# Attention scores as four 64 by 64 products a unit over 192 of 256 keys, with one bias table for all later query tiles

## The reference

```python
scores = scale * np.matmul(q, k.transpose(0, 1, 3, 2))     # 2 batches, 8 heads, 768 rows, 64 wide
is_global = pos[None, :] < int(n_global)                   # 8 keys
is_local = (rel >= 0) & (rel < int(n_local))               # 96 keys
...
scores = np.where(keep, scores + bias, -1000000000.0)
a = np.exp(scores - np.max(scores, axis=-1, keepdims=True))
a = a / (np.sum(a, axis=-1, keepdims=True) + 1e-09)
return np.matmul(a, v)
```

## Time and profile before

| | us |
|---|---|
| the profiled execution, its device time | 368.6 |
| its span (first to last instruction on the core) | 366.7 |
| outside the span | 1.9 |
| median of the three timed executions | 368.89 |

### The profile page before, as it was taken

One profiled execution on the slowest core, in us unless ns is written; L12 is line 12 of the kernel. 1 busy time (PEld: TensorE's weight loads), 2 busy tenths in 40 slices (PEclk: granted clock), 3 DMA queues, 4 the chain that ended last, 5 costly groups with the idle time before them and its releaser, 6 DMA issues.

```text
span 366.7 us, 6163 instructions
## 1 busy us (share of the span) xinstructions
PE 358.0 (98%) x2272; PEld 325.0 (89%) x2272; DVE 215.3 (59%) x574; ACT 177.9 (49%) x450; POOL 91.2 (25%) x168
## 2 busy tenths in 40 slices
PE   7999999999999999999999999999999999999994
PEld 3568898999899999999989999998999999998883
DVE  7886787777777498699785861114853444440000
ACT  3887667677766489663463732113653111112221
POOL 7899786444444200000030300003400000000000
PEclk9999999999999999999999999999999999999999
DMA  7961322333314024213000000000341000002222
GB/s 219 395 218 66 95 95 86 122 133 114 114 45 150 10 65 138 86 59 114 2 0 0 3 0 0 2 32 14 113 131 44 0 2 0 2 0 88 86 87 92
DMA packets 12085, 27.70 MB, mean 76 GB/s; under 512 B 1552, under 2 KB 3984, under 8 KB 12048
## 3 DMA queue, kind: packets, MB, share of 16 engines
q1 hardware_dynamic: 11760, 27.10, 21.8%
q10 hardware_dynamic: 288, 0.13, 0.2%
HBM read 24.08 MB, written 3.15 MB: 74 GB/s over the span
## 4 chain that ended last, share of the span: by engine, by line
PE 93%; DVE 4%; DMA 1%; issue 1%; ACT 0%; POOL 0%; DVEq 0%
PE bank L1570 20%; PE bank L1572 20%; PE bank L1571 20%; PE bank L1534 18%; PE bank L1513 5%; PE bank L1489 5%; PE bank L1444 5%; DVE p_sb L1063 2%; DMA counts<-in_n_keys 1%; DVE xT L1085 0%; DVE denom L1072 0%; DVE table L1040 0%; ACT p_sb L730 0%; DVE pt_sb L1080 0%; ACT out_sb L801 0%
## 5 line engine op out<-in xcount | busy, mean ns | idle before, releaser
L1534 PE MATMUL bank<-xT,w_hi 128*128 128x384 f32 x256 | 69.5, 345 | 0.0
L630 POOL TENSOR_SCALAR p_sb<-p_sb,denom 128x256 f32<-128x256 f32 (+1 forms) x96 | 47.1, 505 | 42.0 <-DVE denom L1074 42.0
L730 ACT ACTIVATE p_sb<-p_sb,row_min 128x256 f32<-128x256 f32 (+1 forms) x96 | 46.3, 486 | 20.9 <-DVE row_min L1063 20.6
L1534 PEld LDWEIGHTS bank<-xT,w_hi 128*128 128x128 f32 x256 | 45.8, 188 | 0.3 <-issue 0.2
L1534 PE MATMUL bank<-xT,w_lo 128*128 128x384 f32 x128 | 44.0, 344 | 0.0
L1570 PE MATMUL bank<-g_hi,w_hi 128*128 128x386 f32 (+1 forms) x128 | 43.3, 338 | 0.0
L1572 PE MATMUL bank<-g_hi,w_lo 128*128 128x386 f32 (+1 forms) x128 | 43.2, 337 | 0.0
L1571 PE MATMUL bank<-g_lo,w_hi 128*128 128x386 f32 (+1 forms) x128 | 43.1, 337 | 0.0
L1100 DVE SCALAR_TENSOR_TENSOR c_sb<-h_sb,conv_sb,c_sb 128x382 f32<-128x382 f32 (+1 forms) x64 | 41.7, 652 | 2.3
L1063 DVE CUSTOM_DVE_ANT_0 p_sb<-bank,table 128x256 f32<-128x256 f32 (+1 forms) x96 | 32.9, 398 | 13.1 <-PE bank L1444 12.7
L651 POOL TENSOR_SCALAR rstd<-mean_var 128x1 f32<-128x1 f32 x12 | 4.7, 391 | 129.2 <-DVE mean_var L1128 129.2
(11 more groups left out here) (96 smaller groups left out, 776.7 us busy)
## 6 DMA issues: line engine op xcount, KB each, us to landing
stage<-in_weights SPq DMA_DIRECT2D x17, 512.0 KB, 3.2
v_sb<-in_v SPq DMA_DIRECT2D x8, 390.0 KB, 3.8
k_sb<-in_k SPq DMA_DIRECT2D x8, 384.0 KB, 3.3
out_dram<-out_sb SPq DMA_DIRECT2D x12, 256.0 KB, 2.2
q_sb<-in_q SPq DMA_DIRECT2D x13, 192.0 KB, 2.4
v_sb<-in_v SPq DMA_DIRECT2D x6, 260.0 KB, 3.2
k_sb<-in_k SPq DMA_DIRECT2D x5, 256.0 KB, 2.7
stage_late<-in_weights SPq DMA_DIRECT2D x2, 512.0 KB, 11.0
```

Of the source, the lines that this page charges most:

```text
L630: nc.gpsimd.tensor_scalar(probs_h, probs_h, denom[:, u % SLOTS, h:h + 1], 1.0, ALU.mult, ALU.mult).then_inc(scaled, 1)
L730: nc.scalar.activation(p_sb[:, u % SLOTS, h, 0:n], p_sb[:, u % SLOTS, h, 0:n], ACT.Exp, bias=row_min[:, u % SLOTS, h:h + 1], scale=-1.0, a ...
L1534: last = nc.tensor.matmul(h_bank(j)[:, 0:C], w, x, start=r == 0, stop=r == F1_GROUP - 1)
```

## The change

Each product is cut into two halves of 64 queries. The keys of a unit now stand as 96 before the tile, 32 first, 128 own, so the first half needs columns 0 to 191 and the second 64 to 255: 192 each. The four products of a unit take the four quarters of the array (two heads by rows, two halves by columns). At `t` = 0 all 128 keys are kept for both halves. The columns that a half leaves out keep what the bank held; the table gives them a value that hides them, and at the start PE writes zeros to the six banks of scores in place of six of the seven warming products. Since `t` = 1 now has its keys in the order of later tiles, one table part serves them all: 384 columns in place of 640, built by DVE alone. The host packs keys and values in the new order (same bytes). DMAs of a second path for wider bands change too; that path does not run with these inputs.

```diff
-WARM = (7, 3, 3, 3)
-TW = 5 * P
+WARM = (1, 3, 3, 3)
+TW = 3 * P
...
-AT_T1, AT_LATER, AT_T0 = 0, 2 * P, 4 * P
+AT_T0, AT_LATER = 0, P
+HALF = P // 2
+NEAR = WK + GK + HALF
...
+SCORE_BANKS = (0, 1, 2, 5, 6, 7)
...
-            nc.gpsimd.iota(rel[:, AT_T0:TW], [[-1, P]], base=0, channel_multiplier=1, **iota).then_inc(consts, 1)
-            nc.gpsimd.iota(rel[:, AT_T1:AT_LATER], [[-1, 2 * P]], base=P, channel_multiplier=1, **iota
...
+            tiles = rel[:, 0:2 * P].rearrange("p (t n) -> p t n", t=2)
+            nc.gpsimd.iota(tiles[:, :, 0:WK], [[P, 2], [-1, WK]], base=-GK, channel_multiplier=1, **iota
...
+            nc.gpsimd.iota(tiles[:, :, WK:P], [[S, 2], [-1, GK]], base=0, channel_multiplier=1, **iota
...
+            nc.gpsimd.iota(rel[:, 2 * P:TW], [[-1, P]], base=0, channel_multiplier=1, **iota).then_inc(consts, 1)
...
-            later = table[:, AT_LATER:AT_T0]
-            pool.wait_ge(tables, COUNT_STEPS)
-            nc.gpsimd.tensor_scalar(later, rel[:, AT_LATER:AT_T0], count_f[:, 1:2], 1.0, ALU.is_ge, ALU.mult
-                                    ).then_inc(later_table, 1)
-            pool.wait_ge(later_table, 1)
-            nc.gpsimd.tensor_tensor(later, later, behind[:, AT_LATER:AT_T0], ALU.add).then_inc(later_table, 1)
...
-            def build_table(at_col, width):
-                cols, near = slice(at_col, at_col + width), table[:, at_col:at_col + GK]
-                link(nc.vector.scalar_tensor_tensor(table[:, cols], rel[:, cols], nl, behind[:, cols], ALU.is_ge,
-                                                    ALU.max))
-                link(nc.vector.tensor_tensor(near, near, reach[:], ALU.min))
+            def build_table():
+                link(nc.vector.scalar_tensor_tensor(table[:], rel[:], nl, behind[:], ALU.is_ge, ALU.max))
+                for at_col in (AT_T0, AT_LATER):
+                    near = table[:, at_col + WK:at_col + P]
+                    link(nc.vector.tensor_tensor(near, near, reach[:], ALU.min))
...
-                at_col = (AT_T0, AT_T1, AT_LATER)[min(t, 2)]
+                at_col = AT_T0 if t == 0 else AT_LATER
...
-            near = table[:, AT_LATER:AT_LATER + GK]
-            dve.wait_ge(later_table, 2)
-            link(nc.vector.tensor_tensor(near, near, reach[:], ALU.min))
...
-            def score(u, h):
+            def score(u, h, half):
                 g, _, hp, tt, t = place(u)
-                n = keys(u)
+                near = slice(0, P) if t == 0 else slice(half * HALF, half * HALF + NEAR)
                 at_key = (0, 0, 2 * P)[t] if t < TG else tt * 2 * P
+                at_query = tt * P + half * HALF
...
-                return nc.tensor.matmul(score_cols(u, h), queries[rows, tt * P:(tt + 1) * P],
-                                        keys_t[rows, at_key:at_key + n], start=True, stop=True)
+                return nc.tensor.matmul(score_cols(u, h)[half * HALF:(half + 1) * HALF, near],
+                                        queries[rows, at_query:at_query + HALF],
+                                        keys_t[rows, at_key + near.start:at_key + near.stop], start=True, stop=True)
...
             def score_unit(u):
-                score(u, 0)
-                return score(u, 1)
+                for half in range(2):
+                    score(u, 0, half)
+                    last = score(u, 1, half)
+                return last
...
+            for i in SCORE_BANKS:
+                nc.tensor.matmul(banks[i][:], zeros[:, 0:P], zeros[:], start=True, stop=True)
             warm(WARM[0])
...
-    band = [np.r_[0:GK, t * P - WK:(t + 1) * P] for t in range(NT)]
+    band = [np.r_[t * P - WK:t * P, 0:GK, t * P:(t + 1) * P] for t in range(1, NT)]
```

More of the change, by code:

```diff
@@ L77 @@
 LEFT2 = NT + 2 * KH + NT
-ALL_DMAS = 11
+ALL_DMAS = 17
 BATCH_STEPS = UNITS * 15
@@ L290, in build_program @@
         tables = sem("tables")
-        later_table = sem("later_table")
         path_in = sem("path_in")
@@ L583, in _ @@
             iota = dict(allow_small_or_imprecise_dtypes=True)
-            nc.gpsimd.iota(rel[:, AT_T0:TW], [[-1, P]], base=0, channel_multiplier=1, **iota).then_inc(consts, 1)
-            nc.gpsimd.iota(rel[:, AT_T1:AT_LATER], [[-1, 2 * P]], base=P, channel_multiplier=1, **iota
+            tiles = rel[:, 0:2 * P].rearrange("p (t n) -> p t n", t=2)
+            nc.gpsimd.iota(tiles[:, :, 0:WK], [[P, 2], [-1, WK]], base=-GK, channel_multiplier=1, **iota
                            ).then_inc(consts, 1)
-            nc.gpsimd.iota(rel[:, AT_LATER:AT_LATER + GK], [[-1, GK]], base=S, channel_multiplier=1, **iota
+            nc.gpsimd.iota(tiles[:, :, WK:P], [[S, 2], [-1, GK]], base=0, channel_multiplier=1, **iota
                            ).then_inc(consts, 1)
-            nc.gpsimd.iota(rel[:, AT_LATER + GK:AT_T0], [[-1, 2 * P - GK]], base=P - GK, channel_multiplier=1, **iota
-                           ).then_inc(consts, 1)
+            nc.gpsimd.iota(rel[:, 2 * P:TW], [[-1, P]], base=0, channel_multiplier=1, **iota).then_inc(consts, 1)
             nc.gpsimd.iota(key[:], [[1, GK]], base=0, channel_multiplier=0, **iota).then_inc(consts, 1)
@@ L593, in _ @@
             nc.gpsimd.memset(minus_half[:], -0.5).then_inc(consts, 1)
-            pool.wait_ge(consts, 8)
+            pool.wait_ge(consts, 7)
             nc.gpsimd.affine_select(out=ident[:], in_=ident[:], compare_op=ALU.not_equal, fill=1.0, base=0,
@@ L801, in copy_out @@
                 nc.scalar.copy(out_sb[:, i % 2, :], banks[i % 4][:]).then_inc(left_o, 1)
-            act.wait_ge(consts, 8)
+            act.wait_ge(consts, 7)
             nc.scalar.activation(spare[:], minus_half[:], ACT.Exp, bias=minus_half[:], scale=-1.0)
@@ L917, in general @@
                                           ).then_inc(all_in, 16)
-                        act.dma_start(v_all[:, 0:2, :], v0[pair].rearrange("p (t n) -> p t n", n=2 * DV)[:, 0:2, :]
-                                      ).then_inc(all_in, 16)
+                        act.dma_start(v_all[0:GK, 0, :], v0[pair, WK:P, 0:2 * DV]).then_inc(all_in, 16)
+                        act.dma_start(v_all[GK:P, 0, :], v0[pair, 0:WK, 0:2 * DV]).then_inc(all_in, 16)
+                        act.dma_start(v_all[:, 1, :], v0[pair, :, 2 * DV:4 * DV]).then_inc(all_in, 16)
                         act.dma_start(v_all[:, 2, :], v0[pair, :, 3 * 2 * DV:4 * 2 * DV]).then_inc(all_in, 16)
@@ L925, in general @@
                             rows = slice(h * D, (h + 1) * D)
-                            act.dma_start(k_all[:, h, 0:2 * P], k0[pair, rows, 0:2 * P]).then_inc(all_in, 16)
+                            act.dma_start(k_all[:, h, 0:GK], k0[pair, rows, WK:P]).then_inc(all_in, 16)
+                            act.dma_start(k_all[:, h, GK:P], k0[pair, rows, 0:WK]).then_inc(all_in, 16)
+                            act.dma_start(k_all[:, h, P:2 * P], k0[pair, rows, P:2 * P]).then_inc(all_in, 16)
                             act.dma_start(k_all[:, h, 2 * P:3 * P], k0[pair, rows, 3 * P:4 * P]).then_inc(all_in, 16)
@@ L1022, in _ @@
                                      ).then_inc(slopes_in, 1)
-            dve.wait_ge(consts, 6)
+            dve.wait_ge(consts, 5)
             link(nc.vector.tensor_scalar(ahead[:], rel[:], 0.0, None, ALU.is_lt))
@@ L1168, in split_lo @@
                                         ).then_inc(w_split, 1)
-            build_table(AT_T0, P)
-            build_table(AT_T1, 2 * P)
+            build_table()
             bias_scores(0)
@@ L1547, in _ @@
             warm(WARM[2])
-            pe.wait_ge(consts, 9)
+            pe.wait_ge(consts, 8)
             f1_next = 0
@@ L1807 @@
         "q": np.ascontiguousarray(q),
-        "k0": np.ascontiguousarray(k[..., np.r_[0:2 * P, band[2]]]),
-        "k1": np.ascontiguousarray(k[..., np.concatenate(band[TG:])]),
-        "v0": blocks(np.r_[0:2 * P, band[2]]),
-        "v1": blocks(np.concatenate(band[TG:])),
+        "k0": np.ascontiguousarray(k[..., np.r_[band[0], band[1]]]),
+        "k1": np.ascontiguousarray(k[..., np.concatenate(band[TG - 1:])]),
+        "v0": blocks(np.r_[band[0], band[1]]),
+        "v1": blocks(np.concatenate(band[TG - 1:])),
         "n_keys": np.array([inputs["n_global"], inputs["n_local"]], np.int64),
```

## The result

The changed kernel took 364.16 us (median of four executions, 363.80 to 364.57), the kernel before beside it on the same chip 368.56 us (median of four, 367.60 to 368.95). The ratio is 0.9885 with a 95% interval of 0.9861 to 0.9908: 4.4 us faster, forecast were 4.5. The profiled execution took 363.8 us.

The account below looks back on a forecast made before the run. PE was taken to bound the kernel from 30.2 us, a chain round PE, DVE, ACT and POOL before. −3.3 − 0.6 − 0.4 − 0.2 = −4.5 us from 368.6 gave 364.1, stated as 364.2 us; range 362.8 to 367.2 us.

Parts of the forecast that it names:

- Scores after 30.2 us: Score products of triples 6 to 15: units of 256 keys cost 192 columns, first weight loads get shorter; −3.3 us together.
- The signs that were named: After 30 us: triples of 1.13 and 1.03 us, four score records starting within some 0.03 us, growing lead over before.
- the lower end: Score price after 30.2 us if each product has a quarter of the array, nothing else in the way: −3.3 us.
- Feeding: Rival at score units: eight records are fed no faster than their pitch, units of 256 keys gain nothing; 368.4 us, chance 0.08.
- Rounds: Rival at score units: four quarters do not run at once, a unit takes two rounds; +6.7, 375.3 us, chance 0.09.
- Loads open in every pass: Rival at score units: the open load of 0.05 us comes twice in each unit; 367.6 us, chance 0.03.
- Table: DVE's start: one step of 384 columns and two limits, first bias step at 6.31 us in place of 6.70; −0.4 us.
- the step ahead of unit 2: DVE's limit on POOL's table part falls away, so unit 2's bias follows the reciprocal; −0.2 us.
- Scores on the early chain: Shorter score products of four single units and one triple on the chain before 30 us; −0.6 us, between nothing and 0.9.
- The rival in which the early stage hides its part: Before 30 us DVE, ACT and POOL set the pace, only the later term and part of the start remain; 365.2 us, chance 0.15.

Follow-up runs that it names:

- the 256-column kernel: Changed kernel with four products a unit over all 256 columns in place of 192: 367.44 us, 0.9971 of the kernel before.
- the last two kernels: Changed kernel with DVE's 1e-9 addition left out: 362.52 us; changed kernel with a single unit's addition cut in two steps, one a head: 362.81 us.
- the repeated run: The changed kernel once more, no edit: 364.17 us against 368.18 for the kernel before, ratio 0.9888.
- the kernel by head with two more writes and the queries later: Changed kernel, products ordered by head, two more small DVE writes at the start, POOL scaling the third tile's queries one unit later: 363.73 us, 0.9879.

## Why the prediction was right, and where it was off

**Scores after 30.2 us, −3.3 us: right.** Between f1 and the last `weigh` the difference grew by 3.98 − 0.81 = 3.2 us. By the chain, six triples lost 0.36 us and four 0.26, together 3.2 us. The signs that were named came in: 1.14 and 1.03 us (forecast 1.13 and 1.03), four products that start within 0.02 us, and no wait of PE after 30 us. The choice of the lower end rested on two ways of sharing that were each seen at full speed; together they are at full speed too.

**Rivals.** Feeding is excluded by the 256-column kernel: with the same eight records a unit a triple takes 1.46 us there and 1.14 us here, so the records are not what a unit waits for. Rounds would have made a triple near 2.1 us. Loads open in every pass would have made it some 1.3 us (three units of 0.42); it is 1.14 in either order of the products.

**Table, −0.4 us, and the step ahead of unit 2, −0.2 us: right where they were read.** The first bias step came 0.38 us earlier (the 384 columns took 0.62 us, forecast 0.70; the two limits 0.68, forecast 0.57 with the gap between them). The bias of unit 2 came 0.69 us earlier, 0.31 from the dropped step.

**Scores on the early chain, −0.6 us: the step that was mis-sized.** The start and this term together were to bring f1 to 29.1 us (−1.2); it came to 29.47 (−0.81). The prediction argued that the units' shorter products count because PE idles for DVE and DVE's next step needs their result, and it took DVE's steps as given. They were not. Groups of its 1e-9 steps and of the reciprocals behind them, 8.9 to 30.2 us, before:

```profile
L1072 DVE TENSOR_SCALAR denom<-denom 128x2 f32<-128x2 f32 x14 | 3.9, 280 | 0.5 <-ACT p_sb L730 0.4
L1074 DVE RECIPROCAL denom<-denom 128x2 f32<-128x2 f32 x14 | 2.3, 166 | 0.5
```

and after:

```profile
L1071 DVE TENSOR_SCALAR denom<-denom 128x2 f32<-128x2 f32 x13 | 3.9, 304 | 0.5 <-ACT p_sb L726 0.4
L1073 DVE RECIPROCAL denom<-denom 128x2 f32<-128x2 f32 x14 | 2.3, 166 | 0.5
```

The mean of the 1e-9 steps went from 280 to 304 ns. The second window holds one of them less; the same 14 steps add up to 3.92 us before and 4.13 after. A reciprocal of the same size takes 166 ns, beside POOL or not, so by an estimate some 0.114 us a step were waiting already before the change, 14 × 0.114 = 1.6 us in this stage. After the change each of the nine steps over 0.2 us ends within 0.05 us behind the end of one of POOL's instructions. The trace before had this to be read, though no row of it was shown: same engine, same size, 0.17 us in one place and over 0.3 in another. The step at 10.56 us had slipped in before:

```profile
11.22 0.17 DVE L1072 TENSOR_SCALAR denom<-denom 128x2 f32<-128x2 f32 x1
```

Now it stood 0.46 us, and f1 came 0.24 us later than in the kernels where it slips in (23.16 against 22.92). Another 0.11 us went to a wait for ACT. The last single unit ahead of `f1` takes 0.56 us in place of 0.70, but the `weigh` behind it 1.35 us, where the chain before has

```profile
28.70 1.24 PE bank L1513 x20
```

In the changed kernel's `weigh` the weight load of the third unit waits for ACT's copy of the turned probabilities: the load starts at 28.47 us, the copy ends at 28.42. All kernels with products of 192 columns show 1.35 or 1.36 us there. Together this is 0.35 of the 0.37 us by which this stage fell short (f1 was to come 0.8 us nearer to the first bias step, by this term and the step ahead of unit 2, and came 0.43 nearer). With the steps cut in two f1 came at 28.71 us, earlier than the forecast's 29.1. So the mechanism of the early chain was right, and the size off because DVE's steps were held by POOL and PE, at the end, by ACT's copy. That POOL held them is shown by the last two kernels; the split of the 0.37 us is read from the traces, and how much the cut steps would give in the kernel before is not shown.

**The sum.** Forecast −4.5 us; the marks give −4.0 and the repeated run −4.0. The −4.4 of the first comparison came from the four executions of the kernel before, 0.4 us slower than in the repeat. That 364.16 us met the forecast of 364.2 is therefore partly luck: the sum took off 0.5 us too much, from a start that lay some 0.4 us too high. The rival in which the early stage hides its part was true in part: of 1.2 us it hid 0.4.

**What holds DVE.** The Trainium skill, SBUF — State Buffer, section on SBUF's two separate sides, tells of a pair of ports that POOL and DVE share: of a POOL instruction and a DVE one in a mode of two ports, or with two inputs from SBUF, whichever starts first holds the pair for its whole instruction. The trace agrees for the step of two numbers a row, with 14.38 beside 14.36 us, though no row shows the mode of a step. That a step of one number a row passes is not told there; the 0.15 us steps show it.

## What to carry to other kernels

Small products share the array in four quarters as well as in two halves, with the loads hidden, so columns that the mask hides anyway can be left out of a half of the queries; price this by the chain, not by the mean of a record. In a stage where four engines work in a ring, look for one operation with two durations in the timeline before pricing a shorter link: here the longer one ended with another engine's instruction, and moving anything ahead of it shifted who met whom. Here cutting a tiny step in two was worth some third of what the whole change gave.

## What the runs showed of the hardware that I had not expected

- A product for a quarter of the array that is busy does not hold back the next ones for other quarters: 1.16 us in place of 1.14 for a triple with the same quarter twice in a row, first starts 13 ns apart in place of 7 (which quarter a record is for is inferred).
- DVE's addition to 128 by 2 numbers waits for POOL's running instruction (up to 0.55 us, in the kernel by head with two more writes and the queries later, in place of 0.17); the same addition to 128 by 1 does not (0.15), nor does the reciprocal (0.17).
- DVE stood still for 0.20 us in the middle of a bias step, at one place in its program, in all seven profiles with the new table that have DVE's program unchanged up to there; with two instructions more ahead of it, and in the last two kernels, the stop is gone. What it is stays open. Taking it away gave nothing by itself: f1 stands at 22.92 us with it and without, since the step behind it then met POOL (0.49 us in place of 0.17).
- The landing of the last output transfer varies from 2.7 to 3.5 us between executions. Without the addition SyncE waited 3.4 us for it, in two steps 2.9, so the profiled spans of these two (361.4 and 361.2 us) stand in the other order than PE's last records (356.17 and 356.47 us). The medians of the two last kernels lie further below that of the changed one (1.65 and 1.35 us) than their marks at the last record do (1.25 and 0.94); that rest was not traced.
